# Weight columns of the level matmuls in steps 2 and 3: from 112 and 96 to 128

## The reference

```
for t in range(S):
    cur = einsum('bhd,bhe->bhde', u * k[t], v[t])
    y[t] = einsum('bhd,bhde->bhe', r[t], state + cur)
    state = w[t][..., None] * state + einsum('bhd,bhe->bhde', k[t], v[t])
x = y as tokens x 384
h = x @ w_in;  x = (h * clip(h + 3, 0, 6) / 6) @ w_out        # d_ff 2048
out = ((x @ w1) * (x @ w2)) @ w3 @ w_out2                     # d_ff 1024
```

## Time and profile before

| | |
|---|---|
| median of 3 runs | 1022.78 us (1022.17 to 1023.91) |
| profiled execution | 1022.78 us |
| its span, first to last instruction | 1021.0 us |
| mean granted TensorE clock | 0.969 |
| TensorE busy | 945.6 us, 93% |
| VectorE busy | 552.5 us, 54% |
| ScalarE busy | 307.0 us, 30% |
| GpSimd busy | 244.4 us, 24% |

### The profile page before, as it was taken

The page is one execution under the profiler, slowest core; times in us unless marked ns, Lnnn a source line. Parts: engine busy times, 40 slices in busy tenths (PEclk is TensorE's granted clock), DMA queues, the critical chain, the costliest instruction groups (busy, mean ns, idle before and its releaser), DMA issues.

```text
span 1021.0 us, 15635 instructions
## 1 busy us (share of the span) xinstructions
PE 945.6 (93%) x6320; PEld 767.9 (75%) x6320; DVE 552.5 (54%) x743; ACT 307.0 (30%) x502; POOL 244.4 (24%) x209
## 2 busy tenths in 40 slices
PE   2579849998999999999999999999999999999997
PEld 1356547777777877877787787787888888888886
DVE  1884558787877677777777853463222222222221
ACT  0113213424333333333323343453213132313222
POOL 0453335344435353535362500000000000000000
PEclk9779959999999999999999999999999999999999
DMA  9953454544342343434334101331101010100000
GB/s 281 298 165 96 131 159 118 138 112 114 110 116 84 112 132 96 133 78 151 90 109 101 55 17 31 120 114 31 63 0 62 1 62 1 62 1 31 1 31 32
DMA packets 79831, 92.84 MB, mean 91 GB/s; under 512 B 9367, under 2 KB 71822, under 8 KB 79630
## 3 DMA queue, kind: packets, MB, share of 16 engines
q1 hardware_dynamic: 69278, 82.13, 28.1%
q10 hardware_dynamic: 10480, 9.70, 3.5%
HBM read 76.07 MB, written 11.01 MB: 85 GB/s over the span
## 4 chain that ended last, share of the span: by engine, by line
PE 77%; DVE 11%; issue 4%; SPq 3%; ACT 2%; DMA 2%; POOL 1%; ACTq 0%; DVEq 0%
PE ps_acc L1008 9%; PE ps_lv L1036 8%; PE ps_h L1008 8%; PE ps_h L1010 8%; PE ps_h L1009 8%; PE ps_acc L1010 8%; PE ps_acc L1009 8%; PE ps_lv L1009 3%; PE ps_lv L1010 3%; PE ps_lv L1008 3%; PE ps_h L1144 3%; DVE k_sb L754 2%; DVE r_sb L754 2%; PE ps_att L1070 2%; DVE totals L754 2%
## 5 line engine op out<-in xcount | busy, mean ns | idle before, releaser
L559 ACT ACTIVATE g_hi<-gated 128x512 fp32r<-128x512 f32 x144 | 90.9, 631 | 395.6 <-DVE gated L902 262.7
L509 POOL TENSOR_TENSOR tok_a<-tok_a 128x384 f32<-128x384 f32 x120 | 144.0, 1227 | 256.0 <-DMA tok_a<-in_k 256.0
L1036 PEld LDWEIGHTS ps_lv<-r_sb,k_sb 48*128 48x128 f32 (+3 forms) x1792 | 94.4, 179 | 59.4 <-issue 46.0
L1036 PE MATMUL ps_lv<-r_sb,k_sb 48*128 48x64 f32 (+3 forms) x1792 | 101.9, 266 | 36.5 <-DVE A_own L824 23.6
L990 DVE TENSOR_TENSOR gated<-gated,ps_lv 128x512 f32<-128x512 f32 x48 | 33.1, 689 | 189.2 <-PE ps_lv L1010 189.2
L910 DVE TENSOR_TENSOR g_lo<-gated,g_hi 128x512 fp32r<-128x512 f32 x96 | 80.0, 833 | 87.5 <-ACT g_hi L559 87.5
L1008 PE MATMUL ps_acc<-g_hi,w_out_hi 128*128 128x512 f32 x288 | 122.2, 424 | 0.0
L1008 PE MATMUL ps_h<-x_hi,w_in_hi 128*128 128x512 f32 x288 | 115.5, 401 | 1.9 <-DVE gated L902 1.8
L1009 PE MATMUL ps_h<-x_hi,w_in_lo 128*128 128x512 f32 x288 | 114.7, 398 | 0.0
L1010 PE MATMUL ps_h<-x_lo,w_in_hi 128*128 128x512 f32 x288 | 114.7, 398 | 0.0
L1009 PE MATMUL ps_acc<-g_hi,w_out_lo 128*128 128x512 f32 x288 | 114.4, 397 | 0.0
(11 more groups left out here) (96 smaller groups left out, 1574.1 us busy)
## 6 DMA issues: line engine op xcount, KB each, us to landing
tok_a<-in_r SPq DMA_DIRECT2D x85, 192.0 KB, 3.0
tok_a<-in_w SPq DMA_DIRECT2D x42, 192.0 KB, 3.7
v_sb<-in_v SPq DMA_DIRECT2D x12, 384.0 KB, 3.6
x_scratch<-x_out SPq DMA_DIRECT2D x6, 768.0 KB, 4.1
x_in<-x_scratch SPq DMA_DIRECT2D x6, 768.0 KB, 6.0
out<-x_out SPq DMA_DIRECT2D x6, 768.0 KB, 3.8
tok_a<-in_k SPq DMA_DIRECT2D x22, 192.0 KB, 4.2
w3T_sb<-in_w3T ACTq DMA_DIRECT2D x8, 512.0 KB, 19.7
```

Of the source, the lines that this page charges most:

```text
L509: return nc.gpsimd.tensor_tensor(dst, x, y, ALU.mult)
L559: return nc.scalar.activation(dst, src, ACT.Copy, **scale)
L1036: last = nc.tensor.matmul(psum[0:count, h, first:first + C // 2] .rearrange("s (n l) -> s n l", l=size), k_g[rows, cols.start:cols.start + ...
```

## The change

Steps 2 and 3 load all 128 columns of k as weights in each matmul, and so write 128 rows of PSUM. Step 4 has 64 columns as before. The added output rows (112 to 127, and 96 to 127) are not read.

```diff
@@ level_products(p, step), L1029
                 k_g, r_g, psum = flat(k_sb[p % 2]), flat(r_sb[p % 2]), banks_of(p, step)
-                count = C if step < MASKED else C - size
+                count = C // 2 if size == C // 2 else C
                 for c in range(2):
                     for a in range(PAIRS):
```

## The result

| | before | after |
|---|---|---|
| median | 1023.35 us (1021.83 to 1025.26, 6 runs) | 1035.17 us (1032.82 to 1038.52, 6 runs) |
| ratio, with its 95% interval | | 1.0114 (1.0089 to 1.0139) |
| profiled execution, its span | 1022.78, 1021.0 us | 1038.02, 1036.2 us |

The kernel became slower, as forecast, but by 11.8 us and not by 8.6, and 1035.2 lies above the range (1028.3 to 1034.0). A second measurement beside the experiments gave 1036.45 us and 1.0125 (1.0103 to 1.0148). The profiled execution is one of the longer ones: 1038.02 us, 15.2 above the profiled one of before.

A forecast was written before the change was run, and what follows sets the result against it. TensorE was taken to bound the kernel: 1022.78 us plus 5.76 (groups 3 to 11), 1.52 (groups 0 and 1) and 1.33 (group 2) made 1031.39, called 1031.4 us. The range was 1028.3 to 1034.0.

The forecast's parts named there:

- Columns, dense part: Groups 3 to 11: wider weights add 0.21 us to step 2 and 0.43 to step 3, 5.76 us in all.
- Head and group 2: Groups 0 to 2: wider steps, some at the low clock, add 1.52 us (groups 0 and 1) and 1.33 (group 2).
- the bound below: Head: if the clock rises when it does now, group 0's step 2 costs 0.21, not 0.45; the sum becomes 8.4 us.
- Waits: From 235 us on: TensorE's waits for VectorE's masked copy (L824) stay at about 5 us and absorb nothing.
- The clock: Whole kernel: the sum left the granted clock as profiled, 1.00 throughout the dense part, and added no time for it.
- falls: Granted clock going from 1.00 to 0.50 and back, behind waiting level steps; the sum added none, priced at 1.6 us each.
- Rival A: Behind waits and level steps: clock falls and rises shift; one fall less gives 1029.8 us, one more 1033.0; chance 0.21.
- A's far end: One clock fall more, and a rise before the first MLP passes later by 2.2 us: 1035.2 us; chance 0.02.
- the two signs of being wrong: Steps read above 1.93 us; or they read 1.93 and the span grows by clearly less than 8 us.
- Theory 1: From the experiments: columns cost as forecast; the remainder is clock falls behind waiting steps 2, as wait plus level matmuls lengthened.
- Theory 3: From the experiments: the clock falls are chance and no more frequent than before.
- Theory 2: From the experiments: the clock falls come from the shift of all later work, whichever step is widened.

The follow-up runs named there:

- after again: The changed kernel, 128 columns in steps 2 and 3 of all groups, measured a second time beside the experiments: 1036.45 us, ratio 1.0125.
- dense only: Against the kernel before, 128 columns in steps 2 and 3 of groups 3 to 11 only: 1030.90 us, ratio 1.0072.
- step 2 only: Against the kernel before, 128 columns in step 2 of all groups, step 3 stays at 96: 1027.58 us, ratio 1.005.
- step 3 only: Against the kernel before, 128 columns in step 3 of all groups, step 2 stays at 112: 1029.12 us, ratio 1.0067.
- head only: Against the kernel before, 128 columns in steps 2 and 3 of groups 0 to 2 only: 1025.93 us, ratio 1.0016.
- long without wait: Against the kernel before, old columns; from group 3 on step 3 issues 14 of its 16 matmuls twice: 1034.54 us, ratio 1.0118.
- same length: Against the kernel before, old columns; from group 3 on the last pair's two matmuls of step 2 are issued twice: 1026.63 us, ratio 1.0034.
- long behind wait: Against the kernel before, old columns; from group 3 on step 2 issues its second chunk's 8 matmuls twice: 1034.27 us, ratio 1.0118.
- project first: From group 3, project matmuls ahead of steps 2, 3, 4 and TURN: changed kernel 1019.66 us, kernel before 1011.29; ahead of step 2 alone, kernel before: 1012.44.

## Why the prediction was wrong

- **Columns, dense part: right.** 5.76 us worked out; 5.6 in the rest of the kernel with the dense part alone, and steps of 1.93 or 2.00 us throughout.
- **Head and group 2: perhaps too high.** 2.85 worked out; 1.4 measured by the means, 0 to 3.3 by the interval. The sum added the low-clock prices, 0.45 and 0.88, and the steps took them (3.70 and 3.68 for 3.25 and 2.82). That a step which grows while the clock is low leaves fewer matmuls for the low clock, the bound below, would explain a smaller sum, but is not shown: behind group 0's step 2 the executions differ by more than these sums (3.95 to 5.42 us for the same eight matmuls).
- **Waits: right.** They stayed, at 5.4 us for 5.0.
- **The clock: the step that failed.** The sum had the granted clock as it was and put falls at nothing. Rival A named the mechanism, the place (a wait, then level matmuls) and the price (1.6; measured 1.55), but allowed one fall more, and had just 0.21 of the chances, one fall less among them. The profiled execution has five more in the dense part. The runs of the second measurement have on average 13.8 us more at the low clock, by the half 6.9 us of time, which with a rest of 5.8 is the 12.7 us between the means; the eleven executions listed with the result have 74.6 us, where before has 62 to 65.
- **Why it was put at nothing**: I had argued that of nine waits from 150 us on only one had a fall. That was one execution, at the old lengths, and the wait of group 4's step 0 at 233.45, ahead of the row that I read from 235 on, was not among them; five of the other profiles have a fall there. The width of the range came from three runs within 0.9 us of their median; the later runs of the same kernel go from 1019.12 to 1028.42 us.
- **Luck**: A's far end, 1035.2, is the measured median, 1035.17. It was reached by one fall and a rise later by 2.2 us, with a chance of 0.02; measured were five falls and first MLP passes that stay low for one pass more (151.71 to 157.12 us; before, 150.68 to 155.24). The number agrees by accident. And the two signs of being wrong that were named, steps above 1.93 us and a span that grows by less than 8, both stayed away.

Over the one profiled execution of each of the 13 kernels, the dense part (groups 4 to 11) has these falls behind a level step that had waited:

| | behind step 2 | behind steps 0 and 1 |
|---|---|---|
| step 2 of 1.93 us (after, after again, dense only, step 2 only) | 11 of 22 | 4 of 12 |
| step 2 of 1.72 us (before, step 3 only, head only, long without wait) | 1 of 21 | 0 of 10 |
| step 2 of 1.92 or 2.57 us at 112 columns (same length, long behind wait) | 1 of 9 | 2 of 4 |
| project first (three kernels) | none waited | 5 of 7 |

- **Theory 1** is borne out in part: by the first two rows of the left column (11 of 22 against 1 of 21), by the time at the low clock with long steps behind waits (12.2 us more), and by the falls that go with the waits. It is not all. The third row, steps as long or longer at 112 columns, has only 1 of 9, in two profiles with little time at the low clock. And the right column has falls behind steps that no kernel lengthened: none of 10 in the second row, 11 of 23 in the others. A wait as such can be followed by a fall.
- **Theory 3** falls: the changed kernel has 78.7 us at the low clock and that with long steps behind waits 73.9, where before has 62 to 65 and the kernels with project first 59 to 62. **Theory 2** is not ruled out as a part, and the right column speaks for it: there the steps have the same length in every kernel. But three of the four kernels in the second row shift later work too, and have no fall there, so chance from one execution to the next can't be told from it. Step 3 alone has 4.2 us more at the low clock with no longer step 2.
- **Open**: what decides at which wait a fall comes, and how much of the increase is length and how much is shift. The sum of step 2 alone (6.3) and step 3 alone (4.2) is below both together (13.8 us), but within the standard errors of 2 us each. The dense part alone has only 3.7, and these 10 us less are three standard errors. Whether the longer steps of the head matter for falls further on, no run shows; by themselves they bring 0.3.

## What to carry to other kernels

Where the engine that bounds the kernel has to wait, and small matmuls follow the wait, a change that lengthens these matmuls can cost twice, as it did here: by itself, and by matmuls at the lower clock behind it. From group 3 to 11 of the profiled execution these are 5.12 and 7.75 us. Read the granted clock behind each such place over several executions, and not in one profile. A wait ahead of small matmuls may be worth filling with large ones that are ready: the order alone, with nothing else changed, made this kernel 1.3% faster (ratio 0.9874), more than the columns cost it.

## What was not expected of the hardware

- The same instructions behind nearly the same wait (0.65 and 0.66 us, then 2.00 us of step 2) were followed by 3 us at the low clock in group 6 and by none in group 5 of one execution (352.42 and 302.88).
- 2.7 us of level matmuls without a wait ahead (60 records, weights of 96 columns) were never followed by a fall in the dense part of that profile (eight places).
- Executions of one program differ by up to 12.5 us, and the time at the low clock goes with it, though not with all of it: for step 2 only, 1023.3 and 1023.4 us with 63 and 61 us at the low clock, 1029.8 and 1035.8 us with 80 and 81.
